# First tiles of a layer norm centred from their sum, and the order of the work around them

## What is computed

```python
for t in range(S):
    kt, vt, rt = (k[:, :, t], v[:, :, t], r[:, :, t])
    cur = np.einsum('bhd,bhe->bhde', u[None] * kt, vt)
    y[:, :, t] = np.einsum('bhd,bhde->bhe', rt, state + cur)
    state = w[None, :, :, None] * state + np.einsum('bhd,bhe->bhde', kt, vt)
...
mu = np.mean(x, axis=-1, keepdims=True)
var = np.mean((x - mu) ** 2, axis=-1, keepdims=True)
xn = (x - mu) / np.sqrt(var + 1e-06) * g_ln
ch = np.maximum(xn @ w_ch1, 0.0) @ w_ch2
x = x + ch
```

## Time and profile before

| | us |
|---|---|
| median of three runs | 387.48 (387.35 to 387.98) |
| the profiled execution, whole | 387.74 |
| its span, first to last instruction | 385.9 |
| outside the span | 1.84 |

### The profile page before, as it was taken

How to read it: one execution, slowest core, us unless ns; L and a number is a source line. 1 busy time by engine, 2 the same in 40 slices (tenths; PEclk the granted TensorE clock), 3 DMA queues, 4 the chain that set the end, 5 groups by cost and what they waited for, 6 DMA issues and landing times.

```text
span 385.9 us, 8882 instructions
## 1 busy us (share of the span) xinstructions
PE 373.9 (97%) x3071; PEld 339.4 (88%) x3071; DVE 278.7 (72%) x612; ACT 156.0 (40%) x283; POOL 136.5 (35%) x114
## 2 busy tenths in 40 slices
PE   8999999999999999999999999999999999999993
PEld 6889988999999999999999655799999999999982
DVE  7798869897998898766668659697656764638440
ACT  6547312312231321241342254378525852555530
POOL 2989772931760480100004005403332233223231
PEclk9999999999999999999999999999999999999999
DMA  7997533400511330500019494799784288111011
GB/s 213 318 314 221 179 141 109 114 20 22 162 54 42 109 109 34 172 3 20 22 50 318 120 304 151 246 370 324 268 322 127 107 254 303 42 34 42 26 45 44
DMA packets 32778, 56.67 MB, mean 147 GB/s; under 512 B 3277, under 2 KB 20339, under 8 KB 32608
## 3 DMA queue, kind: packets, MB, share of 16 engines
q1 hardware_dynamic: 30432, 49.84, 39.5%
q0 software_dynamic: 2304, 6.30, 5.2%
HBM read 51.41 MB, written 5.51 MB: 147 GB/s over the span
## 4 chain that ended last, share of the span: by engine, by line
PE 89%; DVE 4%; DMA 3%; issue 2%; ACT 1%; POOL 0%; SPq 0%; DVEq 0%; POOLq 0%
PE bank L1035 18%; PE bank L935 7%; PE bank L937 7%; PE bank L936 6%; PE bank L1362 5%; PE bank L1334 5%; PE bank L1370 5%; PE bank L1366 5%; PE bank L1338 5%; PE bank L1341 5%; PE bank L1351 3%; PE bank L1263 3%; PE bank L1240 3%; DMA arena<-in_k_t 3%; PE bank L981 2%; PE bank L950 2%
## 5 line engine op out<-in xcount | busy, mean ns | idle before, releaser
L1035 PE MATMUL bank<-xnT_hi,parts 128*128 128x256 f32 x432 | 65.4, 287 | 1.8 <-DVE parts L1563 1.5
L1035 PEld LDWEIGHTS bank<-xnT_hi,parts 128*128 128x128 f32 x432 | 56.6, 191 | 3.8 <-DVE parts L1563 1.7
L731 ACT ACTIVATE parts<-bank 128x512 fp32r<-128x512 f32 x36 | 21.5, 596 | 90.3 <-PE bank L1035 90.3
L1672 DVE SCALAR_TENSOR_TENSOR stage<-stage 128x384 f32<-128x384 f32 x72 | 54.2, 793 | 0.1
L665 POOL DMA_INDIRECT out_y<-late x14 | 20.9, 1489 | 93.5 <-DVE late L1954 93.5
L935 PE MATMUL bank<-parts 128*128 128x384 f32 x144 | 49.3, 342 | 0.0
L937 PE MATMUL bank<-parts 128*128 128x384 f32 x144 | 48.3, 335 | 0.0
L936 PE MATMUL bank<-parts 128*128 128x384 f32 x144 | 48.2, 334 | 0.0
L811 ACT ACTIVATE parts<-stage (+1 forms) x32 | 46.1, 1485 | 0.4 <-DMA stage<-in_w 0.3
L1923 DVE TENSOR_TENSOR parts<-stage,parts x24 | 41.1, 1755 | 5.3 <-ACT parts L811 4.7
L1035 PE MATMUL bank<-xnT_lo,parts 128*128 128x256 f32 x216 | 37.3, 282 | 0.0
(11 more groups left out here) (257 smaller groups left out, 730.6 us busy)
## 6 DMA issues: line engine op xcount, KB each, us to landing
stage<-in_w SPq DMA_DIRECT2D x36, 768.0 KB, 7.8
stage<-in_w_ch SPq DMA_DIRECT2D x6, 768.0 KB, 9.7
arena<-in_k_t SPq DMA_DIRECT2D x12, 224.0 KB, 3.8
arena<-in_r_t SPq DMA_DIRECT2D x12, 224.0 KB, 3.0
arena<-in_v_rows SPq DMA_DIRECT2D x12, 192.0 KB, 4.1
arena<-in_k_rows SPq DMA_DIRECT2D x12, 192.0 KB, 3.3
x_rows<-stage SPq DMA_DIRECT2D x12, 192.0 KB, 1.9
arena<-in_r_rows SPq DMA_DIRECT2D x10, 192.0 KB, 3.4
```

Source lines behind the costliest of these rows:

```text
L731: act.activation(hT_hi[:, 2 * q:2 * q + 2, :].rearrange("p a t -> p (a t)"), bk[6 + q % 2][:], ACT.Relu).then_inc(h_hi_ready, 1)
L1035: mm = pe.matmul(acc, w[:, k, at], x[:, k, :], start=start and k == 0, stop=stop and k == KD - 1, skip_group_check=first and q == 0)
L1672: dve.scalar_tensor_tensor(spent[n % NSPENT], x2[t % 2], 1.0, wgr[:, e * DM:(e + 1) * DM], ALU.mult, ALU.mult, accum_out=lg[:, t, e:e + 1] ...
```

## The change

For the first two tiles the step that makes `mean0` goes. ACT centres with the row sum itself as bias and -384 as scale, so that the tile is 384 times what it was (sum minus 384 x), and the evictions of the two turned tiles use a new column `ngcol0`, the negated gain divided by 384, which POOL makes with one more instruction.

The coefficients of chunk 1 move ahead of the second half of chunk 0's products on TensorE (into another bank, with a wait on the copy that empties it), and ahead of the second half of the masking on DVE. On POOL `diagonal(1)` moves ahead of the gain columns. On ACT both centrings come first, then the rounding of the first half of piece 0, then the eviction of tile 1, then the rounding of the second half, then piece 1.

```diff
             diagonal(0)
+            diagonal(1)
             pool.wait_ge(s_g, 16)
+            pool.tensor_scalar(ngcol0[:], gcol[:], -1.0 / DM, None, ALU.mult)
             pool.tensor_scalar(ngcol[:], gcol[:], -1.0, None, ALU.mult).then_inc(s_ng, 1)
-            diagonal(1)
...
             def first_centred(u):
-                act.wait_ge(s_mean0, u + 1)
-                act.activation(xn[u], tile_of(u), ACT.Identity, bias=mean0[:, u:u + 1], scale=-1.0).then_inc(xn_ready, 1)
+                act.wait_ge(x_ready, u + 1)
+                act.activation(xn[u], tile_of(u), ACT.Identity, bias=sum0[:, u:u + 1],
+                               scale=-float(DM)).then_inc(xn_ready, 1)
...
+                gain = ngcol0 if isinstance(g, int) and g == 0 else ngcol
...
-            round_first(0)
             for u in range(2):
                 first_centred(u)
-            round_first(1)
+            round_first(0)
             act.wait_ge(s_ng, 1)
             turned_tile(0, 1)
+            round_first(1)
             round_piece(1)
...
             scores(1, 1, bk[6:8])
+            pe.wait_ge(s_endS, 1)
+            coefs(1, bk[2])
             first_scores(0, bk[4], scT[0], 1)
-            coefs(1, bk[0])
...
-                dve.wait_ge(x_ready, c + 1)
-                dve.tensor_scalar(mean0[:, c:c + 1], sum0[:, c:c + 1], 1.0 / DM, None, ALU.mult).then_inc(s_mean0, 1)
...
-            masked(1, bk[6:8], scT[1])
-            first_coefs(1, bk[0])
+            masked(1, bk[6:8], scT[1], range(1))
+            first_coefs(1, bk[2])
+            masked(1, bk[6:8], scT[1], range(1, 2))
```

More of the change, by code:

```diff
@@ L157, in build_program @@
         mv = sb("mv", [P, B, 2])
-        sum0, mean0 = sb("sum0", [P, B]), sb("mean0", [P, B])
+        sum0 = sb("sum0", [P, B])
+        ngcol0 = sb("ngcol0", [P, KD])
         vare, root, rstd0, sq, rstd = (sb(n, [P, NT]) for n in ("vare", "root", "rstd0", "sq", "rstd"))
@@ L282, in build_program @@
         s_pair, s_k1, s_hi0, s_wc = sem("s_pair"), sem("s_k1"), sem("s_hi0"), sem("s_wc")
-        s_mean0, s_k2, s_gr, s_spent = sem("s_mean0"), sem("s_k2"), sem("s_gr"), sem("s_spent")
+        s_k2, s_gr, s_spent = sem("s_k2"), sem("s_gr"), sem("s_spent")
         s_v = [sem(f"s_v{u}") for u in range(2)]
@@ L724, in turned_tile @@
                     i = act.activation(xnT_hi[:, k, u * P:(u + 1) * P], bk[u][:, k * P:(k + 1) * P], ACT.Copy,
-                                       scale=ngcol[:, k:k + 1])
+                                       scale=gain[:, k:k + 1])
                 i.then_inc(xnT_hi_ready, 1)
@@ L1538, in first_turned @@
                 for k in range(KD):
-                    i = dve.tensor_scalar(xnT_hi[:, k, 0:P], bk[0][:, k * P:(k + 1) * P], ngcol[:, k:k + 1], None,
+                    i = dve.tensor_scalar(xnT_hi[:, k, 0:P], bk[0][:, k * P:(k + 1) * P], ngcol0[:, k:k + 1], None,
                                           ALU.mult)
@@ L1543, in first_turned @@
                 for k in range(KD):
-                    i = dve.scalar_tensor_tensor(xnT_lo[:, k, 0:P], bk[0][:, k * P:(k + 1) * P], ngcol[:, k:k + 1],
+                    i = dve.scalar_tensor_tensor(xnT_lo[:, k, 0:P], bk[0][:, k * P:(k + 1) * P], ngcol0[:, k:k + 1],
                                                  xnT_hi[:, k, 0:P].bitcast(F32), ALU.mult, ALU.subtract)
@@ L1550, in turned @@
             def turned(g, tiles=range(2)):
+                scale = ngcol if g else ngcol0
                 for u in tiles:
@@ L1554, in turned @@
                     for k in range(KD):
-                        i = dve.scalar_tensor_tensor(xnT_lo[:, k, at], bk[u][:, k * P:(k + 1) * P], ngcol[:, k:k + 1],
+                        i = dve.scalar_tensor_tensor(xnT_lo[:, k, at], bk[u][:, k * P:(k + 1) * P], scale[:, k:k + 1],
                                                      xnT_hi[:, k, at].bitcast(F32), ALU.mult, ALU.subtract)
```

## The result

The changed kernel takes 388.53 us (median of 20 runs), the kernel before, run beside it, 387.08 us (20 runs): ratio 1.003, 95% interval 1.0018 to 1.0043. So it is slower by 0.3%, 0.7 to 1.7 us. The single times of a kernel fall into two groups whose middles are 1.3 to 1.5 us apart (386.2 to 386.8 and 387.4 upwards before, 387.4 to 387.5 and 388.4 upwards after, each group about half of the runs), so that a median of few runs can jump from one to the other, while the fastest execution of each kernel is the steadier measure: 386.16 before, 387.35 after. The profiled execution took 388.40 us with a span of 386.6. Its TensorE clock is at 2.4 GHz as before (0.997 granted), and TensorE's longest wait is still the low part in group 1.

What follows compares the result with a forecast made beforehand. TensorE, its matmuls busy 97% of the span, was taken to bound the kernel. 385.9 span + 0.25 = 386.15, + 1.84 outside = 387.99, less 0.26 to the median gives 387.73; range 386.9 to 388.4.

Steps and rivals of the forecast that it cites:

- TensorE bounds, and the low part in group 1 is where a shift counts: TensorE's matmuls busy 97% of the span; its largest wait, 1.5 us at 58.61, is for DVE's low part.
- The start of group 0, about unchanged: TensorE's start of group 0 at 17.0 to 17.1 against 17.00; bounds 0.5 sooner and 0.3 later.
- The added column hidden in POOL's wait for coefficients: On POOL before its first half: the added column costs 0.23 but replaces a wait, so the first half comes unchanged.
- POOL's second half late by 0.8: The second rounding, behind tile 1's eviction, ends near 17.75, so POOL's second half starts at 17.8 instead of 17.00.
- Who pays, DVE by 0.77: DVE's L1441 at 18.14 waits for POOL's second half; L1442 ends at 22.44 instead of 21.67, 0.77 later.
- POOL covered by its wait for a DMA until 22.18: POOL loses nothing after its third half: free at 21.9, where it stood until 22.18 for a DMA before.
- The turns at 26 and 32 us: DVE's subtraction falls behind POOL's L548; POOL goes first near 32 and leaves group 0 about 0.2 late.
- Rival 1: From DVE's residual at 51.52 to the low part, small steps keep their own lengths: +0.8, 388.3; chance 0.17.
- Nothing behind 58.6: Behind 58.61 TensorE is dense, its other waits each smaller, so the end moves by the low part's +0.25.

Runs made afterwards that it cites:

- the edit of its order: Kernel before with group 1's first low part made by DVE ahead of the five gate products instead of behind them: 385.46 us, ratio 0.9959.
- second trace of before: The kernel before run once more for its trace, no edit: 387.54 us (one run).

## Why the prediction was right or wrong

The sign and the first place were right, the size and the way there were not. The forecast was +0.25 us; measured is +1.2 (0.7 to 1.7), the median of 388.53 lies 0.13 above the upper end, and a kernel that is measurably slower had been given 0.13. That the first two profiles differ by 0.38 at the low part, near the forecast, is luck: the trace of before had a DMA wait that covered the rest. Step by step:

- **TensorE bounds, and the low part in group 1 is where a shift counts.** Held. It was also the larger find: the edit of its order is worth 1.6 us.
- **The start of group 0, about unchanged.** Mis-sized. It is 0.43 later than in the second trace of before (0.19 against the first). The busy matmuls did begin 0.43 later, as their place behind the products says, but the trace that I read had its first rounding held by a late DMA, and with it ACT's centring; in the other trace the transposes follow the busy matmuls at once, so the whole delay passes. By itself it costs nothing at the low part, but in the changed kernel it makes the second rounding late, for which POOL then stood 0.42; that is 0.4 of the loss.
- **The added column hidden in POOL's wait for coefficients.** Wrong, though not what made the loss. I took the place of the old column, and put the new one into 0.1 us of wait. But the change moves the diagonal that had waited ahead of both columns, and POOL's keys' ends start 0.32 later than before, counted from the first diagonal (2.32 against 2.00). In the changed kernel that is covered: the first rounding ends at 15.65 and would hold the first half anyway, and behind it POOL stands for the second rounding.
- **POOL's second half late by 0.8.** Held: 0.95 (17.95; 0.85 counted from the first diagonal). That DVE and POOL exclude each other for whole instructions held as well: in the changed kernel POOL's second half ends 1.69 behind DVE's decay, the next decay 0.55 behind that, POOL's third half 1.70 behind that, with 1.72 and 0.55 in the working. By the Trainium skill (SBUF — State Buffer, section "SBUF: two separate sides") whoever starts first gets the pair of ports. The trace agrees on the exclusion, but not on that reading of "first": POOL's record starts at 17.95, DVE's at 17.96, and DVE went first. The same 0.01 and the same order stand in all five kernels with the moved roundings, so the starts of two records don't tell whose request came first.
- **Who pays, DVE by 0.77.** Wrong, and the step on which the rest hangs. The DMA that had set L1441 to 18.14 came sooner, DVE took the turn, and POOL lost: its third half ended at 22.58, not 21.89. DVE's decays ended at 20.88, not 22.44. TensorE's scores of chunk 2 did come at 22.36, near the 22.5 forecast, but by luck: TensorE had stood 0.42 for POOL's second half and was not waiting for a decay.
- **POOL covered by its wait for a DMA until 22.18.** Wrong for most executions: other traces of POOL on time have 0.17 to 0.92 of that 1.05, or none. Where it is missing, POOL has no cover, and its delay at that point is 1.36 (21.18 to 22.54). This is the difference between 0.38 and 0.93 at the low part.
- **The turns at 26 and 32 us.** Reversed. I had DVE first before and POOL first after. POOL is first in the second trace of before (25.41 against 25.52), and DVE first after, so POOL's L549 ends at 28.81 and its L573 at 34.62, where before L548 ended at 26.41 and L572 at 32.22. Most of those 2.4 us comes back, since before POOL's next instruction stood behind the same subtraction of DVE instead; at the low part of piece 4, 0.89 is left. It is this figure that arrives: 0.89 when POOL enters group 1 (44.00 to 44.89), 0.93 at the low part.
- **Rival 1, the slip passes whole, 388.3.** Near in time, but not by its mechanism. It wanted the chain from the residual to the low part to keep its own lengths. These are POOL's turns: L1676 takes 1.33 behind POOL's L562 as L1672 took 1.34. Against the second trace of before the residual is 0.75 later (51.15 to 51.90), POOL's ends 0.93 (54.05 to 54.98), DVE's first gate product 0.92 (54.15 to 55.07) and the low part 0.93: the chain followed POOL, not the residual.
- **Nothing behind 58.6.** Wrong by 0.35: the wait near 217 us, which no list of what was added or moved would have shown.

At the low part the moved roundings account for 0.45 to 0.5 of the 0.93, and the coefficients, through the eviction that the second rounding stands behind, for the other 0.4. Behind it some 0.3 to 0.4 comes from DVE's shorter list.

## What to carry to other kernels

Where two engines exclude each other by the instruction, a delay of some tenths of a us can change who goes first (here at 26 us, where 0.1 lay between the two in one trace of before) and cost one of them the rest of the other's instruction; forecast both orders, and give them the chances. A wait for a DMA in one trace is no cover until a second execution of the same kernel shows it. Changes that are free or small one at a time can meet: moving work behind an instruction makes it inherit every delay of that instruction. And look at the largest wait of the bounding engine before reordering anything ahead of it: what it waited for stood behind five instructions that could come later.

## What the runs showed of the hardware

Two instructions fewer in DVE's list (610 recorded in place of 612), and the two waits ahead of them, put 0.41 us of standing in front of one instruction 200 us later, with nothing recorded in between, in all four kernels with the shorter list (0.37 in one of them), and none in the two whose list was made up to length again. What makes DVE stand at that place was not shown. The landing of the first piece of W1, seen in the start of ACT's first rounding, differed by 1.2 us between two executions of the kernel before (13.02 and 11.82). POOL's first diagonal, ahead of which POOL's list is the same in all kernels here, came anywhere between 11.25 and 11.71 us; a variant must be compared from a common row, not from zero.
